# Who splits queries and keys: two low halves on GpSimd, one operand by DMA copy, weight low parts on VectorE

## What is computed

```python
# batch 4, heads 8, seq 576, head_dim 64: 32 heads in all
scores = scale * q @ k.T                      # scale = 1/8
bias = -(cum[:, None] - cum[None, :])         # cum = cumsum(max(s, 0))
scores = where(causal, -1e9, scores + minimum(bias, 0))
attn = exp(scores - max(scores)); attn = attn / (sum(attn) + 1e-9)
x = (attn @ v), heads laid side by side       # 2304 x 512
h = x @ w_in                                  # 512 -> 1024
x = layernorm_without_shift(h * softmax(h)) * g_ln @ w_out
out = max(x @ w1, x @ w2, x @ w3) @ w_out2    # 512 -> 768 -> 512
```

## Time and profile before

| | us |
|---|---|
| median of 3 runs | 743.62 |
| lowest, highest | 743.26, 746.23 |
| the profiled execution | 741.23 |
| its span | 739.4 |

### The profile page before, as it was taken

How to read it: one execution, slowest core, us unless ns; L and a number is a source line. 1 busy time by engine, 2 the same in 40 slices (tenths; PEclk the granted TensorE clock), 3 DMA queues, 4 the chain that set the end, 5 groups by cost and what they waited for, 6 DMA issues and landing times.

```text
span 739.4 us, 12543 instructions
## 1 busy us (share of the span) xinstructions
PE 708.7 (96%) x4248; PEld 658.9 (89%) x4248; DVE 391.4 (53%) x700; ACT 320.7 (43%) x765; POOL 254.3 (34%) x284
## 2 busy tenths in 40 slices
PE   3899999999999979999999999999999999999998
PEld 3788998888887878989898999989999899899996
DVE  7999999999958555363535346403213132032120
ACT  3898999888864434242523424112112121121211
POOL 8776789989889363433101000000000000000000
PEclk9999999999999999999999999999999999999999
DMA  6577777768673070900000031010010000100101
GB/s 183 165 205 223 189 202 187 199 179 227 152 166 70 2 156 16 245 12 1 1 1 0 1 114 58 1 43 0 1 43 1 29 14 1 43 0 0 43 0 43
DMA packets 57718, 59.47 MB, mean 80 GB/s; under 512 B 23060, under 2 KB 44692, under 8 KB 57652
## 3 DMA queue, kind: packets, MB, share of 16 engines
q1 hardware_dynamic: 57684, 59.02, 29.7%
HBM read 44.15 MB, written 10.10 MB: 73 GB/s over the span
## 4 chain that ended last, share of the span: by engine, by line
PE 74%; DVE 8%; issue 5%; DMA 4%; POOL 4%; ACT 3%; SPq 1%; DVEq 0%; POOLq 0%; ACTq 0%
PE ps L673 10%; PE ps L674 10%; PE ps L672 10%; PE ps L591 4%; PE ps L590 4%; PE ps L592 4%; PE ps L483 4%; PE ps L517 3%; PE ps L519 3%; PE ps L689 3%; PE ps L688 3%; PE ps L518 3%; PE ps L687 3%; DMA qk_raw<-in_qk_dram 3%; DVE nmax L1084 2%
## 5 line engine op out<-in xcount | busy, mean ns | idle before, releaser
L674 PE MATMUL ps<-x_lo,w_hi 128*128 (+1 forms) x432 | 144.4, 334 | 0.0
L672 PE MATMUL ps<-x_hi,w_hi 128*128 128x384 f32 x432 | 144.3, 334 | 0.0
L673 PE MATMUL ps<-x_hi,w_lo 128*128 128x384 f32 x432 | 144.3, 334 | 0.0
L872 ACT ACTIVATE probs<-ps,nmax 128x576 f32<-128x576 f32 (+4 forms) x160 | 82.6, 534 | 6.5 <-DVE nmax L1084 6.5
L483 PE MATMUL ps<-ident,probs 128*128 128x128 f32 x480 | 75.7, 282 | 9.5 <-DVE pt_lo L1091 6.4
L1091 DVE TENSOR_TENSOR pt_lo<-ps,pt_hi 128x512 fp32r<-128x512 f32 (+1 forms) x128 | 78.2, 652 | 6.7 <-ACT pt_hi L882 3.0
L672 PEld LDWEIGHTS ps<-x_hi,w_hi 128*128 128x128 f32 x432 | 81.1, 188 | 0.2
L673 PEld LDWEIGHTS ps<-x_hi,w_lo 128*128 128x128 f32 x432 | 81.1, 188 | 0.2
L674 PEld LDWEIGHTS ps<-x_lo,w_hi 128*128 128x128 f32 x432 | 81.1, 188 | 0.0
L882 ACT ACTIVATE pt_hi<-ps 128x512 fp32r<-128x512 f32 (+1 forms) x128 | 69.7, 573 | 12.2 <-PE ps L483 10.0
L465 PE MATMUL ps<-k_a,q_a 128*128 128x288 f32 (+2 forms) x192 | 62.7, 334 | 12.1 <-POOL qk_b L745 10.8
(11 more groups left out here) (100 smaller groups left out, 1458.5 us busy)
## 6 DMA issues: line engine op xcount, KB each, us to landing
qk_raw<-in_qk_dram SPq DMA_DIRECT2D x32, 576.0 KB, 4.5
xT<-halves SPq DMA_DIRECT2D x32, 144.0 KB, 2.4
xb_dram<-halves SPq DMA_DIRECT2D x32, 144.0 KB, 2.4
xb<-xb_dram SPq DMA_DIRECT2D x24, 192.0 KB, 3.7
rinvB<-rsum_dram SPq DMA_DIRECT2D x24, 192.0 KB, 4.6
stage<-in_moe_w_dram SPq DMA_DIRECT2D x18, 256.0 KB, 4.4
out_dram<-stage SPq DMA_DIRECT2D x18, 256.0 KB, 2.0
v_raw<-in_v_dram SPq DMA_DIRECT2D x32, 128.0 KB, 3.7
```

Source lines behind the costliest of these rows:

```text
L672: pe.matmul(dst, w_hi[f][:, i, c, :], x2_hi[par][:, c, :], start=(c == 0), stop=False)
L673: pe.matmul(dst, w_lo[f][:, i, c, :], x2_hi[par][:, c, :], start=False, stop=False)
L674: mm = pe.matmul(dst, w_hi[f][:, i, c, :], x2_lo[:, c, bass.ds(g * GT, GT)], start=False, stop=(c == KC - 1))
L872: act.activation(dst, SCORES[c], ACT.Exp, bias=nmax[par][:, c:c + 1], accum_out=sums_all[:, c, bass.ds(t, 1)]).then_inc(exp_done, 1)
```

## The change

It has four parts.
1. GpSimd no longer writes q_b. The upper 64 rows of q_b are filled by a DMA, `copy_q`, that copies q_hi from q_a. It stands at the head of `reload(t)`, for head t-1, and waits there for `q_hi_ready` of that head. For head 0 it stands among the first loads, for head 31 behind the wait for the stores of the reciprocals.
2. q_low moves from VectorE to GpSimd. So that it is a plain subtraction, the lower rows of q_a hold q unscaled, and the lower rows of k_a hold k times the scale; the scale comes as an operand with one value for each row (`q_scale`, `k_scale`, set once by VectorE). GpSimd's `qk_low` subtracts for q, waits for that, and subtracts for k.
3. The low parts of W_in move from GpSimd to VectorE (`win_low`).
4. W_in is split in 16 pieces of 256 columns, one a slot, in the pairs 6 to 13, instead of 8 of 512, one a pair, in the pairs 7 to 14.

```diff
+            def copy_q(h, par):
+
+                sp.wait_ge(q_hi_ready, h + 1)
+                sp.dma_start(f32(q_b[par][0:D, PAD:SP]), f32(q_a[par][0:D, PAD:SP])).then_inc(aux_loaded[par], 16)
...
             sp.wait_ge(rows_zeroed, 2)
+            copy_q(0, 0)
             sp.wait_ge(cum_ready, 2)
...
             def reload(t, par, known=None):
+                copy_q(t - 1, 1 - par)
                 sp.wait_ge(k_hi_ready, t - 1)
                 sp.wait_ge(q_lo_ready, t - 1)
                 sp.wait_ge(k_lo_ready, t - 1)
...
             sp.wait_ge(rinv_stored, 16 * NCH)
+            copy_q(HEADS - 1, 1)
             load_rinv(0)
...
-                pe.wait_ge(aux_loaded[par], (t - par) * 8 + 16)
+                pe.wait_ge(aux_loaded[par], (t - par) * 16 + 32)
...
-                pool.tensor_scalar(q_a[par][:, PAD:SP], q_raw[par][:, :], SCALE, 1.0, ALU.mult, ALU.mult).then_inc(q_hi_ready, 1)
-                pool.tensor_scalar(k_a[par][:, :], k_raw[par][:, :], 1.0, 1.0, ALU.mult, ALU.mult).then_inc(k_hi_ready, 1)
-                pool.tensor_scalar(q_b[par][0:D, PAD:SP], q_raw[par][0:D, :], SCALE, 1.0, ALU.mult, ALU.mult)
-
-            def k_low(t, par):
+                pool.tensor_scalar(q_a[par][:, PAD:SP], q_raw[par][:, :], q_scale[:, :], 1.0, ALU.mult, ALU.mult).then_inc(q_hi_ready, 1)
+                pool.tensor_scalar(k_a[par][:, :], k_raw[par][:, :], k_scale[:, :], 1.0, ALU.mult, ALU.mult).then_inc(k_hi_ready, 1)
+
+            def qk_low(t, par):
+                pool.wait_ge(q_hi_ready, t + 1)
                 pool.wait_ge(k_hi_ready, t + 1)
+                pool.tensor_tensor(q_a[par][D:P, PAD:SP], q_raw[par][D:P, :], f32(q_a[par][D:P, PAD:SP]), ALU.subtract).then_inc(q_lo_ready, 1)
+                pool.wait_ge(q_lo_ready, t + 1)
                 pool.tensor_tensor(k_b[par][0:D, :], k_raw[par][0:D, :], f32(k_a[par][0:D, :]), ALU.subtract).then_inc(k_lo_ready, 1)
...
             def split_win(piece):
...
                 pool.tensor_tensor(hi, raw, one[:, :].broadcast_to([P, WPIECE]), ALU.mult).then_inc(win_hi_ready, 1)
-                pool.wait_ge(win_hi_ready, piece + 1)
-                pool.tensor_tensor(lo, raw, f32(hi), ALU.subtract).then_inc(win_lo_ready, 1)
...
-            with pool.Fori(FIRST, HEADS // 2 - 1) as pair:
+            with pool.Fori(WFIRST, WFIRST + WPIECES // 2) as pair:
                 t = 2 * pair
                 slot(t, 0, None)
+                split_win(t - 2 * WFIRST)
                 slot(t + 1, 1, None)
-                split_win(pair - FIRST)
+                split_win(t + 1 - 2 * WFIRST)
...
-                if live(known, -1):
-                    q_low(t + 1, 1 - par)
...
+            def win_low(piece):
+
+                raw, hi, lo = [w[:, bass.ds(piece * WPIECE, WPIECE)] for w in (stage, *win_flat)]
+                dve.wait_ge(win_hi_ready, piece + 1)
+                dve.tensor_tensor(lo, raw, f32(hi), ALU.subtract).then_inc(win_lo_ready, 1)
```

More of the change, by code:

```diff
@@ L104, in attention_and_mlp @@
         one = sb(keep, "one", [P, 1])
+        q_scale = sb(keep, "q_scale", [P, 1])
+        k_scale = sb(keep, "k_scale", [P, 1])
         x_ = ExitStack()
@@ L183, in attention_and_mlp @@
         rows_zeroed = sem("rows_zeroed")
+        scales_set = sem("scales_set")
         setup_dve = sem("setup_dve")
@@ L266, in attention_and_mlp @@
         block = ctx.enter_context(nc.Block())
-        WPIECES = 8
+        WPIECES = 16
         WPIECE = KC * FF // WPIECES
@@ L270, in attention_and_mlp @@
         RTURN = HEADS - 4
+        WFIRST = HEADS // 2 - 2 - WPIECES // 2
         AHEAD = 2
@@ L752, in _ @@
             pool.wait_ge(rows_zeroed, 2)
+            pool.wait_ge(scales_set, 2)
             pool.sem_inc(pool_passed, 1)
             qk_high(0, 0, 0)
-            k_low(0, 0)
+            qk_low(0, 0)
             pool.wait_ge(setup_pool, 7)
             def split_win(piece):
-                raw, hi, lo = [w[:, bass.ds(piece * WPIECE, WPIECE)] for w in (stage, *win_flat)]
+                raw, hi = [w[:, bass.ds(piece * WPIECE, WPIECE)] for w in (stage, win_flat[0])]
                 pool.tensor_tensor(hi, raw, one[:, :].broadcast_to([P, WPIECE]), ALU.mult).then_inc(win_hi_ready, 1)
-                pool.wait_ge(win_hi_ready, piece + 1)
-                pool.tensor_tensor(lo, raw, f32(hi), ALU.subtract).then_inc(win_lo_ready, 1)
             def slot(t, par, known):
@@ L768, in slot @@
                     qk_high(t + 1, 1 - par, None if known is None else known + 1)
-                    k_low(t + 1, 1 - par)
+                    qk_low(t + 1, 1 - par)
                 if live(known, 1):
@@ L776, in _ @@
                 slot(t, t % 2, t)
-            FIRST = HEADS // 2 - 1 - WPIECES
-            with pool.Fori(2, FIRST) as pair:
+            with pool.Fori(2, WFIRST) as pair:
                 t = 2 * pair
@@ L783, in _ @@
             pool.wait_ge(aux_stored, 16)
-            with pool.Fori(FIRST, HEADS // 2 - 1) as pair:
+            with pool.Fori(WFIRST, WFIRST + WPIECES // 2) as pair:
                 t = 2 * pair
                 slot(t, 0, None)
+                split_win(t - 2 * WFIRST)
                 slot(t + 1, 1, None)
-                split_win(pair - FIRST)
+                split_win(t + 1 - 2 * WFIRST)
+            for t in range(2 * WFIRST + WPIECES, HEADS - 2):
+                slot(t, t % 2, t)
             def join(g):
@@ L1055, in _ @@
         def _(dve):
+            for lo, hi, scale in ((SCALE, 1.0, q_scale), (1.0, SCALE, k_scale)):
+                dve.memset(scale[0:D, :], lo)
+                dve.memset(scale[D:P, :], hi).then_inc(scales_set, 1)
             for row in one_rows:
@@ L1072, in _ @@
             ms.then_inc(setup_dve, 1)
[L1074 to L1079, removed]
             def row_max(t, par, c):
@@ L1100, in invert_sums @@
                 dve.reciprocal(flat, flat).then_inc(rinv_done, 1)
-            q_low(0, 0)
             for i in range(2):
@@ L1140, in _ @@
                 slot(t, t % 2, t)
-            with dve.Fori(2, HEADS // 2 - 2) as pair:
+            def win_low(piece):
+                raw, hi, lo = [w[:, bass.ds(piece * WPIECE, WPIECE)] for w in (stage, *win_flat)]
+                dve.wait_ge(win_hi_ready, piece + 1)
+                dve.tensor_tensor(lo, raw, f32(hi), ALU.subtract).then_inc(win_lo_ready, 1)
+            with dve.Fori(2, WFIRST) as pair:
                 t = 2 * pair
@@ L1144, in _ @@
                 slot(t + 1, 1, None)
+            with dve.Fori(WFIRST, WFIRST + WPIECES // 2) as pair:
+                t = 2 * pair
+                slot(t, 0, None)
+                win_low(t - 2 * WFIRST)
+                slot(t + 1, 1, None)
+                win_low(t + 1 - 2 * WFIRST)
+            assert WFIRST + WPIECES // 2 == HEADS // 2 - 2
             for t in range(HEADS - 4, HEADS):
```

## The result

| | before | after |
|---|---|---|
| median, us (17 runs each) | 743.47 | 748.85 |
| lowest, highest | 741.68, 746.3 | 746.5, 753.43 |
| ratio, 95% interval | | 1.008 (1.0064 to 1.0095) |
| the profiled execution, its span | 741.23, 739.4 | 750.2, 748.4 |

The changed kernel is slower by 0.8%. The forecast was 751.3 us with a range of 739.5 to 763; the sign and the size were right, the size in part by luck, as the account of the terms shows.

What follows compares the result with a forecast made beforehand. TensorE and VectorE were both taken as near their limit at 6.16 us a slot. W_out +3.0, W_in +4.7, start-up +2.0 and end -2.0 made +7.7 on 743.62: 751.3 us, range 739.5 to 763.

Steps and rivals of the forecast that it cites:

- The ring: Attention stage: load lands, q_hi runs, SyncE waits for it, copies, issues the next load; 1.72 us plus landing per head.
- The turn with L: One turn of each pair: the ring's 1.72 us plus the load's landing behind the pair's W load.
- L: Landing time of the q and k load: 4.0 us without W ahead, 4.8 behind W_out, 5.5 behind W_in.
- The SyncE turn: The pair's other turn, SyncE's issuing from copy to copy with W in it: 7.00 us for W_in, 6.46 for W_out.
- start-up: First heads: GpSimd does head 0 in a row, so the load of head 2 goes out later, +2.0 us.
- three W_in pairs: Pairs with W_in loads after the start-up: 13.9 us a pair against 12.33, three times 1.57, +4.7 us.
- W_out stretch: Eight pairs with W_out loads: 12.7 us a pair against 12.33, eight times 0.37, +3.0 us.
- end: Last four heads wait for few loads and VectorE lacks q_low: four times 0.5 us, -2.0 us.
- this rival: Attention stage: GpSimd becomes the bound, slots with a W piece near 6.5 us, +5 us, 748.6 us; chance 0.04.
- The slot in which nothing is late: Attention stage without q_low on VectorE: 5.7 to 5.9 us a head against 6.16, worth 6 to 12 us.
- the first rival: Attention stage: loads keep ahead and the relief shows, 5.8 us a slot, 735.6 us, 739.6 at half relief; chance 0.18.
- The signs that I had named: Expected in the profile after: waits of q_hi and SyncE, slot lengths, VectorE's share in slices 2 to 10, step after 220 us.

Runs made afterwards that it cites:

- ring_alone: The kernel before, with copy_q at the head of reload and without GpSimd's write of q_b, nothing else moved; 758.59 us, ratio 1.0215 to the kernel before.
- late_small: The changed kernel, copying only 4 of 64 rows of q_hi, behind the loads of q, k and v; 739.92 us, ratio 0.9965 to the kernel before.
- experiment 11: Also head_small_aux_first: the changed kernel with 4 of 64 rows copied and aux right behind the copy, ahead of q and k; 757.49 us, ratio 1.0209.
- new_order: The changed kernel with SyncE issuing q and k, full copy, aux, then W, v, stores; 742.21 us, ratio 0.9985 to the kernel before.
- late: The changed kernel with the full copy moved behind the loads of q, k and v, ahead of aux; 753.61 us, ratio 1.0147 to the kernel before.
- late_vpack: The changed kernel with full copy behind the loads and v laid out for one DMA with rows of 1280 bytes; 758.66 us, ratio 1.0197.

## Why the prediction held, and which terms didn't

**The ring** was the right mechanism in the W_in stretch: the chain shows it link by link. From q_hi of head 2 to that of head 12 the kernel before takes 59.4 us and the changed one 66.3; ring_alone, with the engines' work of before but for the write of q_b, takes 65.4, and late_small, which has neither ring nor bytes, 60.1. So the ring alone gives nearly all of that loss; the wait for aux behind it is part of it (experiment 11). Its size there, 13.9 us a pair forecast, and 15.0, 14.1 and 12.7 measured, 13.9 in the mean, is luck: both turns of the pair were off by 1.1 us, in opposite ways. The turn with L took 8.8, 8.3 and 7.0 us, copy to copy, where I had 6.9; L behind W_in was 6.9, 6.4 and 5.2 us where I took 5.5 less 0.3. The SyncE turn took 6.2 (42.71 to 48.88), 5.8 and 5.7 where I had 7.0.

**Term by term**, in us of lateness of the profiled execution:

| | forecast | measured | where from |
|---|---|---|---|
| start-up | +2.0 | +2.0 | q_hi of head 2 |
| first W_in pair | 0 | +2.0 | head 2 to head 6 |
| three W_in pairs | +4.7 | +5.3 | head 6 to head 13 |
| W_out stretch | +3.0 | -2.2 | head 13 to head 24 |
| reload behind the joined halves | not seen | +1.5 | head 24 to head 30 |
| end | -2.0 | -1.0 | q_hi of head 30 (+8.65) to copy of the halves of head 31 (+7.7) |
| MLPs | 0 | +1.3 | span +9.0 |

Only the start-up came out as forecast, and the W_in pairs within 0.6 us. The W_out stretch had the wrong sign and was 5.2 us off; what I put at nothing or didn't see (2.0, 1.5 and 1.3) made up for most of that. That the total is 9.0 against 7.7 is therefore in good part luck.

*The W_out stretch.* The forecast had 12.7 us a pair, 6.46 for SyncE's turn and 6.5 less 0.3 for the ring's with L = 4.8; measured are 12.0. The loads land in 3.4 to 4.1 us (90 to 175 us), 3.9 in the median. A ring turn is then 1.72 + 3.9 = 5.6, and SyncE's turn with a W load took no more than 6.0 (96.57 to 102.57); both hide behind the 6.0 of GpSimd and TensorE. Two terms failed. L was taken from a row of before in which the W load stood 1.0 us in front; here it stands 1.9 us in front (89.50 to 91.41), and the 0.3 that I took off for that was too little. And SyncE's turn had 1.13 us from aux to the first store; it was 0.72 (99.29 to 100.01). The 13.2 a pair of ring_alone is no support for the forecast, as its L is 3.9 too. The range had a slip as well: it counts L in 22 turns, while its own pairs, eleven of them, have L in one turn each, so 0.3 us of it is 3.3 us and not 6.6.

*GpSimd.* I read its 3.90 busy us from one window and came to 4.5 to 4.7, or 5.3 with a W_in high part. That window, 83 to 89 us, held 3.90 only because it cuts a subtraction at either end (82.43 to 83.85, and from 88.71 on). The means of before add up to 4.53 (0.67 + 0.67 + 0.84 + 1.47, and 0.88 for v). Those of after are 0.74 + 0.75 + 1.42 + 1.45 + 0.88 + 0.61, with the wait of 0.15: 6.00, the measured slot. It didn't stay under 5.9, as I had it; that it still cost nothing is because 6.0 is under 6.16. I gave this rival 0.04. Its subtractions took 1.4 us and not 1.9, so its 6.5 us a slot and its loss aren't there, but a GpSimd without a gap is, level with TensorE in half of the stage. The scale as an operand was costed at 0, within -0.1 to +0.3, and measured +0.07 and +0.08.

*The slot in which nothing is late.* I took 5.7 to 5.9 us. It is 6.0: new_order has TensorE busy in 95.00 of 95.00 us at that pace, and so has late_small. The calm window said so already, 6.00 of 6.00 busy, and I let one short slot outvote it. The relief is thus 0.16 us for each of 26 slots, 4 us, and the start-up eats half of it. No run came near the 735.6 of the first rival; late_small with 739.9 is the most that any gave.

**The end** gave 1.0 in place of 2.0. Ahead of it stands a term that I had not seen at all: the reload of head 29 stands behind the four loads of joined halves. The chain of after at 179 us:
```profile
178.75 0.68 SPq L369
...
180.80 0.62 SPq L369
181.46 0.61 SPq L307
...
183.91 4.24 DMA qk_b<-aux_dram
```
It costs the changed kernel 2.4 us in the halves of heads 24 to 25 (+6.3 to +8.65) and new_order 0.6.

**VectorE's low parts** were costed at 0.7 us each; they took 1.37 beside GpSimd. It cost nothing, because VectorE had the time. That q_low's absence doesn't show is right as a pattern but for another reason than the ring in the W_out stretch: there VectorE is busy for 87.90 of 96 us (84 to 180 us), with GpSimd in front of it at 91.41 and TensorE at 94.26.

**The signs that I had named.** SyncE's wait for q_hi: there. q_hi waiting for its load in nearly every head: only in 11, and in nearly all of them (28) only in head_small_aux_first. Slots near 7 us before 80 us: there. 6.4 after: no, 6.0. VectorE from 9 to 7 tenths: 6 and then 9 again. In step from 220 us on: all but the last 1.3 us; they arise in a stretch in which the granted clock was 0.84 and 0.93 (270 to 300 us) against 0.89 and 1.00 before. No run isolates that, and it stays open.

**Where the full change's loss lies, then.** Taken together, the runs fit this: what counts is what stands in the queue in front of the two transfers that somebody waits for, the load of q and k, and aux. A wait in front of the load (ring) holds up the first; W, q, k, v and copy in front of aux (late) hold up the second. new_order moves both forward and has neither loss. It moves copy, aux, W and v at once, so it shows what the order is worth, and not which of the moves does it. As a gain over the kernel before, nothing is shown: new_order's interval includes 1.

## What to carry to other kernels

Before a wait is put into an in-order issuing queue, list what is queued behind it and who waits for each of these, and order the queue by how soon each transfer is needed: the same transfers in another order were worth 6.6 us here. A small transfer landed later where more had been issued just ahead of it (4.1 us behind 1.2 MB, 5.5 to 7.0 behind 1.4 MB), so count the bytes in front of it and not only its own. Sum an engine's work for one slot from the means of its operations, never from one short window, and take the slot limit from the engine that shows no idle time. When a sum comes out right, check its terms all the same: here two turns were each 1.1 us off and their sum was exact.

## What the hardware showed that I had not expected

- An 18 KB transfer took 6.5 and 7.0 us to land when about 1.4 MB had been issued just before it (late_vpack), and 4.2 us in the changed kernel (38.15 and 183.91).
- GpSimd's one-input pass over 128x576 took 742 and 748 ns with one scale value for each row, 671 with a constant.
- VectorE's one-input pass over 64x576, float32 out of SBUF, took 1404 ns in the mean beside GpSimd's subtractions, and the low part of 128x256 took 1367 or 641 ns depending on what ran beside it. The Trainium skill (SBUF — State Buffer, Who interferes with whom) names the first form as one that can take a two-port mode, and then both engines shut each other out; the 1404 ns agree with that. For the sum it means that a pass moved to VectorE isn't cheap because it has one input.
- The DMA engines moved 246 GB/s in a stretch (new_order) in which 214 had looked like their limit.
